# A scan in two interleaved chains, products of two quarters inside it, and fill matmuls in a fused attention and expert kernel

## The reference

```python
mag = np.sqrt(a_re * a_re + a_im * a_im)
scale = np.minimum(mag, 0.999) / (mag + 1e-06)
a_re_n, a_im_n = (a_re * scale, a_im * scale)
for t in range(S):
    new_re = ar * S_re - ai * S_im
    new_im = ar * S_im + ai * S_re
    S_re, S_im = (new_re + kv, new_im)        # kv = outer(k[t], v[t])
    y[:, :, t] = einsum(q[:, :, t], S_re)
...
x = attn_out.transpose(0, 2, 1, 3).reshape(B * S, H * D)
x = _moe_ref(x, ...)       # argmax gate, capacity 384, relu(x @ w1) @ w2
return (x @ w_a) * (x @ w_b) @ w_out
```

## Time and profile before

| | |
|---|---|
| median of 3 runs | 642.39 us |
| profiled execution | 641.07 us, its span 639.80 us |
| TensorE busy | 556.4 us (87%) |
| VectorE busy | 368.0 us (58%) |
| ScalarE busy | 274.9 us (43%) |
| GpSimd busy | 40.4 us (6%) |
| mean granted TensorE clock | 0.942 of full |

### The profile page before, as it was taken

The page is one execution under the profiler, slowest core; times in us unless marked ns, Lnnn a source line. Parts: engine busy times, 40 slices in busy tenths (PEclk is TensorE's granted clock), DMA queues, the critical chain, the costliest instruction groups (busy, mean ns, idle before and its releaser), DMA issues.

```text
span 639.8 us, 10173 instructions
## 1 busy us (share of the span) xinstructions
PE 556.4 (87%) x3838; PEld 497.0 (78%) x3839; DVE 368.0 (58%) x813; ACT 274.9 (43%) x570; POOL 40.4 (6%) x51
## 2 busy tenths in 40 slices
PE   0546473869999998799999999999999999999996
PEld 0223241769999997699999999788888888888886
DVE  4699999556766665488888888453422222222211
ACT  6545551851222223477777878343423212221112
POOL 1000000000111111600000000000002000020002
PEclk9977775989999997799999999999999999999999
DMA  8980010289221210566666662442001000010001
GB/s 335 392 311 0 1 75 41 108 213 303 65 75 46 75 31 20 183 226 225 210 216 217 203 202 87 148 144 75 1 0 51 0 1 0 1 51 0 1 0 50
DMA packets 42280, 70.09 MB, mean 110 GB/s; under 512 B 13056, under 2 KB 35328, under 8 KB 41536
## 3 DMA queue, kind: packets, MB, share of 16 engines
q1 hardware_dynamic: 40704, 64.80, 30.7%
q0 software_dynamic: 1536, 4.73, 2.3%
HBM read 52.97 MB, written 16.55 MB: 109 GB/s over the span
## 4 chain that ended last, share of the span: by engine, by line
PE 76%; DVE 14%; ACT 4%; DMA 4%; issue 2%; SPq 0%; POOL 0%; DVEq 0%; ACTq 0%; POOLq 0%
PE psum L1171 24%; PE psum L1144 11%; PE psum L969 10%; PE psum L1004 10%; PE psum L780 4%; DVE region L349 4%; PE psum L621 3%; PE psum L756 3%; DVE region L354 2%; PE psum L784 2%; PE psum L797 2%; PE psum L662 1%; DMA x_rows<-queries 1%; PE psum L908 1%; PE psum L264 1%
## 5 line engine op out<-in xcount | busy, mean ns | idle before, releaser
L1186 DVE TENSOR_TENSOR ga<-ga,psum 128x512 f32<-128x512 f32 x36 | 24.8, 688 | 132.6 <-PE psum L1171 132.6
L264 PE MATMUL psum<-region,ident 128*128 128x384 f32 (+1 forms) x42 | 27.1, 740 | 60.4 <-ACT region L273 33.5
L264 PEld LDWEIGHTS psum<-region,ident 128*128 128x128 f32 x42 | 11.5, 294 | 70.9 <-ACT region L375 29.0
L1190 ACT ACTIVATE gh<-ga 128x512 fp32r<-128x512 f32 x36 | 22.8, 632 | 81.9 <-DVE ga L1186 77.3
L969 PE MATMUL psum<-xh,w1h 128*128 128x224 f32 x192 | 53.5, 279 | 1.3 <-DVE xl L918 1.3
L1004 PE MATMUL psum<-hh,w2h 128*128 128x224 f32 x192 | 54.2, 282 | 0.0
L1184 ACT ACTIVATE ga<-psum 128x512 f32<-128x512 f32 x36 | 21.5, 598 | 75.3 <-PE psum L1171 75.3
L969 PE MATMUL psum<-xl,w1h 128*128 128x224 f32 x192 | 53.5, 278 | 0.0
L969 PE MATMUL psum<-xh,w1l 128*128 128x224 f32 x192 | 53.4, 278 | 0.0
L1004 PE MATMUL psum<-hh,w2l 128*128 128x224 f32 x192 | 52.6, 274 | 0.0
L1004 PE MATMUL psum<-hl,w2h 128*128 128x224 f32 x192 | 52.5, 274 | 0.0
(11 more groups left out here) (182 smaller groups left out, 1459.4 us busy)
## 6 DMA issues: line engine op xcount, KB each, us to landing
raw<-w SPq DMA_DIRECT2D x14, 1536.0 KB, 6.8
sorted_x<-region SPq DMA_DIRECT2D x8, 579.0 KB, 10.7
queries<-qk SPq DMA_DIRECT2D x4, 1152.0 KB, 15.8
xrow<-sorted_x SPq DMA_DIRECT2D x7, 579.0 KB, 4.0
region<-x_rows SPq DMA_DIRECT2D x14, 288.0 KB
queries<-w SPq DMA_DIRECT2D x2, 1536.0 KB, 13.6
x_rows<-region SPq DMA_DIRECT2D x5, 576.0 KB, 2.8
region<-a SPq DMA_DIRECT2D x4, 576.0 KB, 7.8
```

Of the source, the lines that this page charges most:

```text
L264: nc.tensor.matmul(x, ident[:], x0[:, cut], start=True, stop=False)
L1186: m = dve.done(tt(ga[f % 2][:], ga[f % 2][:], bb[:, 0:TT], ALU.mult))
L1190: m = act.done(ss.activation(gh[f % GB3][:], ga[f % 2][:], ACT.Copy))
```

## The change

- One DMA brings both planes of a piece of a.
- For pieces 0 and 1 VectorE squares the second plane itself. `newton(0)`, `negated(0)` and the squares of piece 2 are moved forward, and nine scan steps instead of six stand ahead of `newton(2)`.
- A scan step is four instructions: two products of 192 elements (one for each half of the pair), then two sums of 96.
- All products of quarters 0 and 1 stand between quarters 2 and 3 of the scan, their turns on banks 6 and 7.
- The last quarter's squares, sum, Ln and Exp are done in two parts, 8 steps and 4.
- 19 fill matmuls of the identity with itself (`warm`, 128 x 384, result unused), each waiting for a scan step: ten ahead of the sum of quarter 2, six ahead of the first part of the sum of quarter 3, three ahead of its second.
- V of the first batch is loaded after the third inverse instead of the last.
- In unit 0 the y matmuls stand ahead of the state update; the six instructions for Wr and Wi stand behind the scores of units 0 and 1.

```diff
-                for i in range(2):
-                    sp.dma_start(piece(1 + i, n_), a[:, i, lo * PAIR:min(hi * PAIR, SA)]).then_inc(s_a[n_], 16)
+                w = min(hi * PAIR, SA) - lo * PAIR
+                sp.dma_start(walk(AT_Z[1] + lo * PAIR, [SA, 2], [1, w]), a[:, :, lo * PAIR:lo * PAIR + w]
+                             ).then_inc(s_a[n_], 16)
...
-                act.done(ss.activation(T(0, n_), piece(1, n_), ACT.Square))
-                m_sq[n_] = act.done(ss.activation(T(1, n_), piece(2, n_), ACT.Square))
+                m_sq[n_] = act.done(ss.activation(T(0, n_), piece(1, n_), ACT.Square))
+                if n_ >= ON_PE:
+                    m_sq[n_] = act.done(ss.activation(T(1, n_), piece(2, n_), ACT.Square))
...
-                    dve.wait(m_sq[n_])
+                    vv.wait_ge(s_a[n_], 16)
+                    m = dve.done(tt(T(1, n_), piece(2, n_), piece(2, n_), ALU.mult))
+                    dve.wait(m_sq[n_], m)
                     m_x2[n_] = dve.done(tt(T(0, n_), T(0, n_), T(1, n_), ALU.add))
...
-                    m = dve.done(tt(by.rearrange("p (u v c) -> p u v c", u=2, v=2),
-                                    walk(AT_Z[2] + prev, [-SA, 2], [0, 2], [1, PAIR]),
-                                    walk(AT_Z[0] + now, [SA, 2], [SA, 2], [1, PAIR]), ALU.mult))
-                    dve.wait(m)
-                    half = by.rearrange("p (u v c) -> p u v c", u=2, v=2)
-                    m_step[i] = dve.done(tt(walk(AT_Z[1] + now, [SA, 2], [1, PAIR]), half[:, 0], half[:, 1], ALU.add))
-                    dve.wait(m_step[i])
+                    m = []
+                    for k_ in range(2):
+                        if i - 1 in m_step:
+                            dve.wait(m_step[i - 1][k_])
+                        m.append(dve.done(tt(by[k_], walk(AT_Z[2] + prev + k_ * D, [-SA, 2], [0, 2], [1, D]),
+                                             walk(AT_Z[0] + now + k_ * D, [SA, 2], [SA, 2], [1, D]), ALU.mult)))
+                    m_step[i] = []
+                    for k_ in range(2):
+                        dve.wait(m[k_])
+                        m_step[i].append(dve.done(tt(walk(AT_Z[1] + now + k_ * D, [SA, 2], [1, D]),
+                                                     by[k_][:, 0], by[k_][:, 1], ALU.add)))
...
-            def slot_squares(s):
-                act.wait(m_step[TI * (s + 1) - 1])
+            def slot_squares(s, lo=0, hi=3):
+                act.wait(m_step[TI * s + TI // 3 * hi - 1][1])
                 if s == 3:
-                    act.wait(m_kx[2])
+                    act.wait(m_turn[3 * TI // TB - 1])
+                    ss.wait_ge(s_xrows[0], 32)
+                cut = slice(lo * (W // 3), hi * (W // 3))
                 for i in range(2):
-                    m_s2[s] = act.done(ss.activation(B_(s, i), flat(AT_Z[1 + i] + s * W, W), ACT.Square))
-
-            def slot_sum(s):
-                m_sm[s] = sum_on_pe(SETS[s], B_(s, 0), B_(s, 1), W, m_s2[s])
-
-            def slot_inverse(s):
+                    m_s2[s] = act.done(ss.activation(B_(s, i)[:, cut], flat(AT_Z[1 + i] + s * W, W)[:, cut], ACT.Square))
+
+            def slot_sum(s, lo=0, hi=3):
+                m_sm[s] = sum_on_pe(SETS[s], B_(s, 0), B_(s, 1), W, m_s2[s], range(lo, hi))
+
+            def slot_inverse(s, lo=0, hi=3):
+                cut = slice(lo * (W // 3), hi * (W // 3))
                 act.wait(m_sm[s])
-                m = act.done(ss.activation(thirds(B_(s, 0)), sums(SETS[s], W), ACT.Ln))
+                m = act.done(ss.activation(thirds(B_(s, 0))[:, lo:hi], sums(SETS[s], W)[:, lo:hi], ACT.Ln))
                 act.wait(m)
-                m_le[s] = act.done(ss.activation(B_(s, 1), B_(s, 0), ACT.Exp, scale=-1.0))
+                m_le[s] = act.done(ss.activation(B_(s, 1)[:, cut], B_(s, 0)[:, cut], ACT.Exp, scale=-1.0))
...
+            def warm(i):
+                pe.wait(c_id, m_step[i][1], *(free[7] or ()))
+                nc.tensor.matmul(bank[7][:, 0:3 * P], ident[:], ident[:].unsqueeze(1).broadcast_to([P, 3, P]),
+                                 start=True, stop=True)
...
+            newton(0)
             squares(1)
-            newton(0)
...
+            m_one = dve.done(vv.memset(flat(AT_Z[2] + D, D), 0.0))
+            negated(0)
             rsqrt(1)
-            negated(0)
+            squares(2)
+            x2(2)
+            dve.wait(m_one)
+            scan(1, 3)
             weight(1)
-            squares(2)
-            x2(2)
-            scan(1, 2)
+            scan(3, 4)
             scaled(1)
             negated(1)
             rsqrt(2)
-            scan(2, 7)
+            scan(4, 10)
             newton(2)
             weight(2)
-            scan(7, TI)
+            scan(10, TI)
...
-            scan(2 * TI, 3 * TI)
+            scan(2 * TI, 2 * TI + 2)
             scaled(4)
             negated(4)
+            scan(2 * TI + 2, 3 * TI)
+            for i in range(2 * TI, 3 * TI - 2):
+                warm(i)
             slot_inverse(1)
             slot_squares(2)
             inverse_times(0)
             slot_sum(2)
             inverse_times(1)
             slot_inverse(2)
-            for x, n in PLACES[:3]:
+            for x, n in (PLACES[3], *PLACES[:3]):
                 product(0, x, n)
                 turn(0, x, n, (6, 7))
+            for x, n in PLACES:
+                product(1, x, n)
+                turn(1, x, n, (6, 7))
             scan(3 * TI, 4 * TI - 4)
+            for i in range(3 * TI, 4 * TI - 6):
+                warm(i)
+            slot_squares(3, 0, 2)
+            slot_sum(3, 0, 2)
             inverse_times(2)
+            sp.wait_ge(dve.sem, m_kx[2][1])
+            sp.dma_start(flat(AT_V, P // 2 * D, L), v[0]).then_inc(s_v[0], 16)
             scan(4 * TI - 4, 4 * TI)
-            slot_squares(3)
-            slot_sum(3)
+            for i in range(4 * TI - 4, 4 * TI - 1):
+                warm(i)
+            slot_inverse(3, 0, 2)
+            slot_squares(3, 2, 3)
+            slot_sum(3, 2, 3)
+            slot_inverse(3, 2, 3)
 
             tmp = flat(AT_W, 4 * D).rearrange("p (i d) -> p i d", d=D)
             a0 = [flat(AT_Z[1 + i] + HALF * PAIR, D) for i in range(2)]
             lo_at = (HALF - 1) * PAIR
+            dve.wait(*m_step[HALF - 1])
...
-            product(0, *PLACES[3])
-            turn(0, *PLACES[3], (6, 7, 3, 4, 5))
-            for x, n in PLACES:
-                product(1, x, n)
-                turn(1, x, n, (6, 7, 3, 4, 5))
-            slot_inverse(3)
             for x, n in PLACES:
                 product(2, x, n)
                 turn(2, x, n, (6, 7, 3, 4, 5))
             inverse_times(3)
-            sp.wait_ge(dve.sem, m_kx[3][1])
-            sp.dma_start(flat(AT_V, P // 2 * D, L), v[0]).then_inc(s_v[0], 16)
             for x, n in (("x", 0), ("x", 1), ("q", 1), ("q", 0)):
                 product(3, x, n)
             for x, n in (("x", 0), ("x", 1), ("q", 1), ("q", 0)):
-                turn(3, x, n, (6, 7, 3, 4, 5), (1,) if (x, n) == ("q", 0) else ())
+                turn(3, x, n, (6, 7, 3, 4, 5), (0, 2) if (x, n) == ("q", 0) else ())
...
+            pool.wait(m_kx[3])
             m_set = pool.done(g.memset(flat(AT_SC, 2 * YB * L, L), 0.0))
-            dve.wait(m_eT)
...
-            dve.done(tt(Wi[:, 0:P - 1], Wi[:, 0:P - 1], ws[1][:, 0:P - 1], ALU.add))
...
+            sp.wait_ge(dve.sem, m_kx[3][1])
...
+                if n == 0:
+                    end_factors()
...
+                if more and n:
+                    state_in()
...
+                    if more and not n:
+                        state_in()
```

44 lines of the change are left out of this document (23 added, 21 removed).

## The result

The changed kernel takes 623.97 us (median of 4 runs, 623.43 to 625.90) and the kernel before, on the same chip, 642.49 (4 runs): ratio 0.9722, 95% interval 0.9683 to 0.9761. Its profiled execution took 623.43 us with a span of 622.2 us at a mean granted clock of 0.969 (before 0.942). The forecast was 624.

The account below looks back on a forecast made before the run. VectorE was taken to bound the kernel up to 145 us, then TensorE; only an earlier start of the unit loop counts. Last inverse 13.2 plus tail 5.2 gave 18.4 us, so 622.7 profiled, 624 as median; range 618 to 632.

Parts of the forecast that it names:

- Head: Stages up to the inverses: piece 2's squares 1.7 us earlier, third Newton step from 28.57 to about 26.8 us.
- Scan step: VectorE's product and sum as two chains: 0.87 us a step instead of 0.98; first inverse at 69.9 us.
- 1.36 us a step: Rival, interleaving doesn't pay: four scan-step instructions each pay the dependent price; 642 us, no change; chance 4%.
- First fills: Ten TensorE matmuls ahead of quarter 2's sum: 6.4 us in a row, sum warm near 76, costing what they save.
- Turns through two banks: 24 turned blocks of quarters 0 and 1: 0.655 us each, four at 0.87; copies end near 98.9 us.
- Last inverse: VectorE's inverse of the last quarter starts at 111.5 us instead of 124.7, 13.2 us earlier.
- Tail: From last inverse into the unit loop: update at +14, unit 0's swap at +15.3 instead of +20.1; 5.2 us gained.
- Sum: Whole kernel: 13.2 + 5.2 = 18.4 us gained, 622.7 on the profiled run's terms, forecast 624.
- rivals: Clock lost in turns 17%, x load still slow 8%, faster turns 7%, interleaving doesn't pay 4%, fills never warming the clock 3%.
- Clock lost in the turns: Rival: waits between turned blocks let TensorE's clock fall, 0.87 us a block instead of 0.655; 631 us; chance 17%.

Follow-up runs that it names:

- e1: Kernel after with the old scan step again (one product of 384, one sum of 192): 624.63 us, ratio 0.9741 to the kernel before.
- e12: Kernel after without the nine fills of the last quarter, the first ten kept: 621.86 us, ratio 0.9702 to the kernel before.
- e5: Kernel before with only the scan step split into two interleaved chains: 636.20 us, ratio 0.9921 to the kernel before.
- e2: Kernel after without all 19 fill matmuls: 620.43 us, ratio 0.9670 to the kernel before.
- e4: Kernel after with the turned blocks of quarters 0 and 1 going round five banks instead of two: 620.53 us, ratio 0.9677 to the kernel before.
- e8: Kernel after with unit 0's state update ahead of its y matmuls and the end factors behind its copy: 625.77 us, ratio 0.9756 to the kernel before.
- e3: Kernel after with V of the first batch loaded behind the last inverse again: 630.73 us, ratio 0.9807 to the kernel before.
- e9: Kernel after run once more, no edit: 623.42 us, ratio 0.9722 to the kernel before.
- e6: Kernel after with the loads of the pieces split in two DMAs again: 623.91 us, ratio 0.9727 to the kernel before.
- e7: Kernel after with five banks for the turns of quarters 0 and 1 and the last quarter in one part: 624.70 us, ratio 0.9746 to the kernel before.

## Why the prediction was right, step by step

The steps came as forecast, each mark within 1.2 us. Two terms were sized right and yet the time hardly needs them: the shorter scan step, which is worth less here than the sum gave it (e1), and the last nine fills, which cost more than they bring (e12). That the median met the forecast to 0.1 us is luck: errors of both signs cancel, and the part behind the swap alone scatters by 3 us. No run undoes the move of the products of quarters 0 and 1 alone, the largest part of the change, nor the reordering of the head, nor the second block that VectorE copies in the last turn; what these are worth is read from the traces only.

- **Head.** Third Newton step at 26.24 to 26.52, forecast 26.8. Nearly all the slack is gone: 0.46 to 0.94 us of wait remain. The squares of piece 2 came 1.4 us earlier (14.50), forecast 1.7. The rest, 0.9 in that trace, came from a side that the prediction did not have: TensorE's sum of piece 2 took 5.8 us up to ScalarE's Ln (16.85 to 22.69) instead of 6.7 (18.25 to 24.97), because its last three matmuls ran at full clock instead of its last two.
- **Scan step.** 0.875 us, forecast 0.87; 26 steps and the work between them took 43.04 us, forecast 43.1. The Trainium skill, VectorE: DVE Perf Modes, section "Rules for kernel authors", says to keep the number of chained operations small rather than their semaphores, since the drain comes regardless. The prediction read that as 1.36 us a step, an estimate. The trace disagrees: a step of four instructions takes 0.875, less than the 0.98 of two. (The prediction gives that case as 641 and as 642 us; its own terms make 642.) In the kernel before the split alone is worth 4.9 us in the medians and 3.9 in "between" (e5); in the kernel after it is worth about 1 (e1): there the turned blocks wait for TensorE's sum and ScalarE's Ln, and the 2.2 us of wait ahead of the last inverse take up most of VectorE's delay. My sum gave the 26 steps their full 2.7 us, and e1 shows that most of this would have been made good without the split.
- **First fills.** "They cost what they save" holds: the sum of quarter 2 is at full clock at 76.00 and the first copy at 82.30, both as forecast, and without them the Ln comes about as early (e2).
- **Turns through two banks.** 0.66 us a block (15.9 us for the 24), forecast 0.655. The four blocks at half clock that I had put in didn't come; the copies end at 98.2 instead of 98.9. This was named as what is late next, and it is: e4 shows that two banks cost about 3 us.
- **Last inverse.** 110.30, forecast 111.5. The turns ended 0.7 us earlier and the 0.9 us for a start at half clock was not needed; 0.4 of this was lost on the way from the last copy to the inverse, 12.1 us instead of 11.7. VectorE would have wanted it at 110.30 - 2.17 = 108.13, forecast 108.1. The sum counted the last nine fills at their length without asking whether they were needed; they cost 1.3 to 1.8 us (e12).
- **Tail.** From the inverse the scores come at +12.1, the update at +14.5 and the swap at +15.9; forecast were 11.4 to 11.7, +14 and +15.3. The 0.6 was there by the update: the scores were 0.4 late. I had put the six end-factor instructions beside unit 0's matmuls; in truth the update's copy stands behind them, from 124.53 to 125.84, but that costs only about 0.1 us: the copy starts 1.01 us behind the start of the update, and 0.89 where nothing stands in front (124.03 and 124.92 in e8). The 5.2 us forecast for the tail were 4.8 up to the swap of unit 0 and 0.4 behind it; 4.2 and 0.6 came. V's move is worth 3.3 of the 4.2: without it the way from the inverse to the swap is 19.3 us instead of 15.9 (e3).
- **Sum.** 18.6 us at the swap of unit 0, forecast 18.0 (the 18.4 of the sum hold 0.4 that lie behind it): the inverse came 1.2 earlier than forecast and the tail took 0.6 longer. At the swap of unit 1 it is 19.2, and what follows gave 1.6 us back in that trace, nearly all of it in the stretch at half clock that e9 does not have. Of the rivals none came. "Clock lost in the turns" failed: through the waits between the blocks, and one of 2.02 us behind the first eight transposes, the clock stayed up (TensorE of after, then the windows over most of the turns):

```profile
82.93 2.51 PE L442 MATMUL psum<-ident,region 128*96 128x128 f32 x16 [2.02 <-ACT region L450]
```
```profile
82.00:90.00 8.00, 6.14 (x43) 4.22 (x44) 7.87 (x17) 6.89 (x13) 0.00 (x0) 1.00 0.55 222
90.00:98.30 8.30, 6.67 (x47) 4.35 (x45) 8.27 (x25) 6.96 (x14) 0.00 (x0) 1.00 0.00 0
```

TensorE is idle for a fifth of these 16 us (the prediction said a third), and the granted clock is 1.00 throughout, where in the kernel before it had been 0.50 at 92 us. There the turns had begun behind a wait of the same length, 2.03 us. In e2, where no fills stand ahead of the turns, the clock stays at 1.00 too. So why it fell in the kernel before is not shown, and neither is why it stayed up here.

## What to carry to other kernels

A chain of dependent short instructions on VectorE is shortened by splitting it into two independent ones of half the width, as long as each reader comes two instructions behind its writer; but it is worth only what no other engine takes over, and that must be read anew once other edits stand beside it (4 to 5 us alone, about 1 in company). Work for TensorE that only keeps its clock up paid nowhere here: ten fills in a gap that was long enough saved 0.4 us at most, within the scatter, and nine ahead of a sum that would otherwise start earlier cost 1.3 to 1.8. When a long stretch is freed by reordering, look next at the number of buffers that the freed work goes round: here two PSUM banks instead of five took back 3 us. A large load in front of a write that someone waits for costs the write about what the load still has to go; move it to where nobody waits behind it.

## What the runs showed of the hardware

- V, 1152 KB, takes 7.4 us from issue to landing in the kernel after and 7.3 in e3. A write of x rows (576 KB) issued 2.5 us behind it takes 7.8 instead of 3.15 us (e3): the delay of 4.7 is about what the load still had to go, 4.8.
- The first reader of piece 0 started at 3.76, 3.77 and 4.42 us in the three traces with two DMAs of 192 KB (before, e6, e5), and at 4.22 to 4.67 in those with one DMA of 384 KB. The start scatters by 0.7 us with two DMAs; that one DMA is later is not shown.
- A pause of 2.2 us did not lower TensorE's granted clock at once but some matmuls later: in e7 the pause ends at 104.30, the next pairs of matmuls start 0.75 us apart, and from 105.80 on they start 1.28 apart.
- The same kernel, in the same place, had a stretch at half clock of about 3 us in one trace (389 to 392 us, after) and none in the next (e9).
- A wait of about 2 us ahead of the turned blocks was followed by a fall of the granted clock in the kernel before (0.50 at 92 us) and by none in the kernel after and in e2.
